# The recurrence of a three-part layer, from chunks of 128 tokens with scores of a whole chunk to sub-chunks of 64 with a running softmax

## The chip, the cores and the metric

One core of one Trainium2 chip. The metric is the device time of one execution in microseconds. A plain run gives 465.87 us (median of three, 465.07 to 466.24).

## The reference, cut to what matters

Batch 4, 8 heads, 768 tokens, head dimension 48; then a soft mixture of 8 experts with 4 slots each over all 3072 tokens (model dimension 384, hidden 1024), then a dense layer 384 to 2048 to 384 with a squared ReLU.

```python
    for t in range(S):
        kt, vt, rt = (k[:, :, t], v[:, :, t], r[:, :, t])
        cur = np.einsum('bhd,bhe->bhde', u[None] * kt, vt)
        y[:, :, t] = np.einsum('bhd,bhde->bhe', rt, state + cur)
        state = w[None, :, :, None] * state + np.einsum('bhd,bhe->bhde', kt, vt)
...
    logits = x @ phi
    d = logits - logits.max(0, keepdims=True)
    d = np.exp(d)
    d /= d.sum(0, keepdims=True) + 1e-09
    slot_input = d.T @ x
...
        h = np.maximum(slot_input[e] @ w1[e], 0.0)
        slot_out[e] = h @ w2[e]
...
    c = logits - logits.max(1, keepdims=True)
    c = np.exp(c)
    c /= c.sum(1, keepdims=True) + 1e-09
    return (c @ slot_out).astype(np.float32)
...
    h = x @ w_in
    r = np.maximum(h, 0.0)
    g = r * r
    return (g @ w_out).astype(np.float32)
```

## The kernel before

The program is written engine by engine: every engine has its own list, in an order written out by hand, and semaphores between them. There is no planner. All data is fp32; a matmul of fp32 stands in the trace as two records.

**Recurrence.** The tokens come in 6 chunks of 128 (`CH`), the heads in 4 pairs (`HP`), and a *unit* is one pair of heads in one chunk, for all 4 batches: 24 units. A pair of heads lies on partitions 0 to 47 and 64 to 111 (`HEAD_ROWS`). In each unit:

- VectorE multiplies the keys with powers of w (`keys`, L638), then the queries, each head on its own 48 partitions into a tile whose other half is zero (`queries`, L644, two instructions), so that one matmul over 112 rows gives the scores of both heads (L865: four matmuls, 256 columns). It carries the state on (`state`, L680), copies the scores above the diagonal over a prepared diagonal (`scores`, L667), sums the bonus term r·u·k (`bonus`, L662) and multiplies the keys in token-first layout (`keys_n`, L653).
- GpSimd makes the products r·k·u (`ruk`, L402, L405) and the diagonal matrices from `bonus` (`scores`, L413, 128x1024).
- TensorE makes scores (L865), output from state and scores (`y_ps`, L887 and L890, 16 matmuls of 128 columns) and the increment of the state (`aux_ps`, L904). In the second unit of a chunk it also does the router for the chunk before: logits (`pair_logits` L839, `token_logits` L854) and x turned to token-first (`turn_x`, L847).
- ScalarE copies out of PSUM (`copy_y` L474, `keep_x` L484, `state_in` L503).

All x (`x_sb`) and all logits are kept. The softmax over tokens comes after the recurrence: maximum of the first five chunks, exponentials, then the gather into slots (L948, 24 tiles), with the last chunk following and a factor that joins both.

**Experts** follow from L997 on (first layer; second layer L1022), then a short part up to `gin`, then the **dense layer**, 96 steps of 12 matmuls (L1081) with 384 columns. Weights come in through the SyncE queue: w1 in 24 pieces beside the recurrence, w2 after it.

The order on an engine is the order of its calls: for VectorE `scale`, `advance`, `mask_scores`, `sum_bonus`, `scale_n`; for TensorE `unit_scores`, `unit_output` of the unit before, `unit_state`.

## Time and profile before

| what | value |
|---|---|
| median of three runs | 465.87 us |
| span of the profiled execution | 464.3 us |
| PE busy | 405.0 us, 87% |
| VectorE busy | 331.9 us, 71% |
| ScalarE busy | 174.4 us, 38% |
| GpSimd busy | 153.1 us, 33% |
| DMA | 60.30 MB, mean 130 GB/s |
| first unit's scores on TensorE | at 11.65 us |
| last output of the recurrence | ends at 178.3 us |
| first matmul of the experts | at 190.56 us |
| dense layer in its steady rhythm | 237.4 to 464.3 us |

The profile is of one execution. Its own time beside the span isn't given apart; the median of the runs is 1.6 us above the span. Busy time of a pipelined engine like TensorE is not its capacity, so the stage must be found first (the windows), and then who is never idle in it.

### The profile page before, as it was taken

The page shows a single profiled execution, that of the slowest core. Times are in us where ns is not written, and L with a number is a line of the kernel's source. Part 1 is how long each engine was busy: PE and PEld are TensorE (multiplying, and loading weights), DVE is VectorE, ACT ScalarE, POOL GpSimd, SP SyncE. Part 2 cuts the span into 40 slices and gives each one's busy share as a digit, 9 for nine tenths or more (in the row PEclk, how much of TensorE's full clock was granted, in tenths as well). Part 3 has the DMA queues.
Part 4 walks back from the last instruction along what each step waited for, and adds up shares of the span by engine and source line. Part 5 has one row for each costly group of instructions (what it writes and reads, how often), then busy time and mean ns, then how long its engine had stood idle before and what let it go on. Part 6 is the DMA issues. An engine that isn't in the chain of part 4 may idle for free.

```text
span 464.3 us, 8783 instructions
## 1 busy us (share of the span) xinstructions
PE 405.0 (87%) x3096; PEld 349.0 (75%) x3096; DVE 331.9 (71%) x439; ACT 174.4 (38%) x312; POOL 153.1 (33%) x111
## 2 busy tenths in 40 slices
PE   0856968778787889999679999999999999999997
PEld 0544857657676766235279999999999999999997
DVE  8599999999999994611596565565556556556553
ACT  2011313123031314012535555555555555555552
POOL 6578878898888850110550000000000000000000
PEclk9957999999998989899889999999999999999999
DMA  6966667667666769999600010001001001001001
GB/s 174 243 195 193 202 206 218 183 201 231 194 196 203 225 238 316 373 373 403 212 0 1 1 68 2 1 1 68 0 0 68 0 0 68 0 0 68 1 0 68
DMA packets 31844, 60.30 MB, mean 130 GB/s; under 512 B 2640, under 2 KB 25296, under 8 KB 31440
## 3 DMA queue, kind: packets, MB, share of 16 engines
q1 hardware_dynamic: 31824, 60.02, 40.9%
q8 instruction: 13, 0.21, 0.2%
q14 instruction: 7, 0.06, 0.1%
HBM read 55.30 MB, written 4.72 MB: 129 GB/s over the span
## 4 chain that ended last, share of the span: by engine, by line
PE 61%; DVE 14%; POOL 10%; issue 5%; DVEq 1%; ACT 1%; POOLq 0%; ACTq 0%
PE out_ps L1081 43%; POOL scores L413 8%; PE h_ps L1059 5%; DVE scores L667 4%; DVE queries L644 4%; PE wide L997 3%; PE wide L1022 2%; PE score_ps L865 2%; DVE bonus L662 1%; DVE state L680 1%; PE y_ps L890 1%; POOL ruk L402 1%; POOL ruk L405 1%; PE wide L948 1%; DVE keys L638 1%
## 5 line engine op out<-in xcount | busy, mean ns | idle before, releaser
L1081 PE MATMUL out_ps<-w_hi,act_hi 128*128 128x384 f32 x384 | 130.5, 340 | 5.2 <-DVE act_lo L819 4.0
L1081 PE MATMUL out_ps<-w_hi,act_lo 128*128 128x384 f32 x384 | 131.0, 341 | 0.0
L1081 PE MATMUL out_ps<-w_lo,act_hi 128*128 128x384 f32 x384 | 130.5, 340 | 0.0
L814 DVE TENSOR_TENSOR act<-relu_h 128x512 f32<-128x512 f32 x96 | 68.2, 711 | 78.3 <-ACT relu_h L576 78.3
L576 ACT ACTIVATE relu_h<-h_ps 128x512 f32<-128x512 f32 x96 | 57.3, 597 | 100.6 <-PE h_ps L1059 97.9
L865 PE MATMUL score_ps<-queries,keys 112*128 112x256 f32 x192 | 60.5, 454 | 29.7 <-DVE queries L644 29.7
L413 POOL TENSOR_TENSOR scores<-ident,bonus 128x1024 f32<-128x1024 f32 x24 | 74.4, 3101 | 23.2 <-DVE bonus L662 23.2
L1081 PEld LDWEIGHTS out_ps<-w_hi,act_hi 128*128 128x128 f32 x384 | 72.7, 189 | 6.2 <-ACT act_hi L579 3.3
L1081 PEld LDWEIGHTS out_ps<-w_lo,act_hi 128*128 128x128 f32 x384 | 72.9, 190 | 3.8
L1081 PEld LDWEIGHTS out_ps<-w_hi,act_lo 128*128 128x128 f32 x384 | 72.5, 189 | 0.0
L819 DVE TENSOR_TENSOR act_lo<-act,act_hi 128x512 fp32r<-128x512 f32 x96 | 68.4, 713 | 4.6 <-ACT act_hi L579 1.0
L865 PEld LDWEIGHTS score_ps<-queries,keys 112*128 112x128 f32 x192 | 39.3, 222 | 41.8 <-DVE queries L644 24.1
L644 DVE TENSOR_TENSOR queries<-rk,q_pow 48x512 f32<-48x512 f32 x48 | 67.4, 1405 | 0.3
L579 ACT ACTIVATE act_hi<-relu_h 128x512 fp32r<-128x512 f32 x96 | 60.9, 634 | 3.9
L474 ACT ACTIVATE x_t<-y_ps 112x512 f32<-112x512 f32 x24 | 14.3, 597 | 111.2 <-PE y_ps L890 111.2
L890 PE MATMUL y_ps<-scores,rkv 128*48 128x128 f32 x384 | 38.0, 286 | 1.8 <-DVE scores L667 1.8
L1059 PE MATMUL h_ps<-mix_t,gin 128*128 (+1 forms) x96 | 38.0, 398 | 0.0
L887 PE MATMUL y_ps<-queries,state 112*48 112x128 f32 x320 | 32.6, 278 | 4.3 <-DVE scores L667 4.1
L667 DVE COPY_PREDICATED scores<-mask,score_ps 128x1024 f32<-128x1024 uint32 x24 | 32.0, 1333 | 4.8 <-POOL scores L413 4.8
L402 POOL TENSOR_TENSOR ruk<-rkv 128x384 f32<-128x384 f32 x24 | 31.0, 1291 | 10.8 <-DMA rkv<-in_rkv_n 8.5
L890 PEld LDWEIGHTS y_ps<-scores,rkv 128*48 128x48 f32 x384 | 24.6, 129 | 4.3 <-DVE scores L667 2.9
L887 PEld LDWEIGHTS y_ps<-queries,state 112*48 112x48 f32 x320 | 18.6, 123 | 10.8 <-issue 7.5
(145 smaller groups left out, 369.1 us busy)
## 6 DMA issues: line engine op xcount, KB each, us to landing
rkv<-in_rkv_n SPq DMA_DIRECT2D x24, 576.0 KB, 4.6
rk<-in_rk_t SPq DMA_DIRECT2D x48, 192.0 KB, 3.2
w_sb<-in_w SPq DMA_DIRECT2D x24, 384.0 KB, 5.1
w_room<-in_w SPq DMA_DIRECT2D x4, 1536.0 KB, 11.1
out_dram<-y_sb SPq DMA_DIRECT2D x5, 768.0 KB, 3.5
w_x<-in_w SPq DMA_DIRECT2D x2, 1536.0 KB, 14.0
w_w<-in_w SPq DMA_DIRECT2D x4, 768.0 KB, 11.5
w_in_sb<-in_w_in SPq DMA_DIRECT2D x3, 1024.0 KB, 13.0
```

The source lines that it names most:

```text
L413: nc.gpsimd.tensor_tensor(scores[hp % 2][:, :, :, :].rearrange("p b h t -> p (b h) t"), ident[:, :].unsqueeze(1).broadcast_to([P, 2 * B, P ...
L576: nc.scalar.activation(relu_h[f % 2][:, :], h_ps[f % 4][:, :], ACT.Relu).then_inc(relu_done, 1)
L579: nc.scalar.activation(act_hi[f % 4][:, :], relu_h[f % 2][:, :], ACT.Square).then_inc(act_hi_done, 1)
L644: last = nc.vector.tensor_tensor(queries[hp][rows, :, half], rk[hp % 2][rows, 0], q_pow[rows, hp].unsqueeze(1).broadcast_to([D, B, P]), AL ...
L667: nc.vector.copy_predicated(scores[hp % 2][:, :, :, :].rearrange("p b h t -> p (b h) t"), mask[:, :].unsqueeze(1).broadcast_to([P, 2 * B, P]),
L814: nc.vector.tensor_tensor(act[f % 2][:, :], relu_h[f % 2][:, :], relu_h[f % 2][:, :], ALU.mult).then_inc(act_done, 1)
L819: nc.vector.tensor_tensor(act_lo[f % 4][:, :], act[f % 2][:, :], act_hi[f % 4][:, :].bitcast(F32), ALU.subtract).then_inc(act_lo_done, 1)
L865: last = nc.tensor.matmul(score_ps[hp % 2][:, 2 * P * b:2 * P * (b + 1)], keys[hp % 2][0:PAIR, b], queries[hp][0:PAIR, b].rearrange("p h t ...
L887: nc.tensor.matmul(y_ps[SECOND * half:SECOND * half + D, cols], state[0:PAIR, hp, b], queries[hp][0:PAIR, b, half], start=True, stop=False)
L890: last = nc.tensor.matmul(y_ps[SECOND * half:SECOND * half + D, cols], rkv[hp][:, 2, b, D * half:D * (half + 1)], scores[hp % 2][:, b, hal ...
L1059: nc.tensor.matmul(h_ps[f % 4][:, :], gin[:, P * f:P * (f + 1)], mix_t[:, bass.ds(g * B, B), :], start=True, stop=True).then_inc(h_mm, 1)
L1081: last = nc.tensor.matmul(out_ps[t][:, 0:DM], a[f % 4][:, tok], w[:, f], start=(f == 0 and i == 0), stop=(f == NF - 1 and i == 2))
```

## The change

The recurrence is written anew and the router is folded into it.

- **Sub-chunks.** A chunk of 128 tokens is two sub-chunks of 64 (`SUBS`), each with its own scores. Keys, queries and values use one half of the array's rows and one half of its columns per matmul: a score matmul reads 48 rows (one head) and 64 key columns, and streams 128 columns: 64 of the queries and 64 of a second set. Sixteen of them make a unit. The state has two versions per unit: `state_a` at the middle of the first sub-chunk, `state_b` at the second (powers of w count from the middle, token 64).
- **Powers.** VectorE multiplies the keys of both heads in one instruction (`times_keys`), GpSimd the queries in one (`times_queries`). The zero-filled queries are gone.
- **Diagonal.** The second set, queries times u·w (ScalarE, `second_queries`), gives the bonus on its diagonal; a second masked copy takes it (`mask_scores`, masks `strict` and `diag`). The GpSimd products, the diagonal matrices and the sum are gone.
- **Keys in token-first layout** aren't loaded and multiplied, but turned from `keys` by TensorE (`turn_keys`) and copied by ScalarE (`copy_keys`). Of the token-first load only the values stay (192 KB for 576).
- **Router.** Logits are made slot-first per chunk (`slot_logits`), the softmax over tokens runs along with a running negative maximum (`new_peaks`, `exponents`), p and logits are turned (`turn_logits`), and the gather of each chunk goes into an accumulator that is rescaled (`gather`, `gathered`). `x_sb` holds one chunk. After the recurrence only the last chunk's share is left, and a factor per batch and slot (`GAIN`, `fold_g`).
- **Weights.** All of w1 and two experts of w2 come in beside the recurrence; four experts of w2 after it instead of six.
- The experts' matmuls and the dense layer are as before, but for where tiles lie; on VectorE one clearing of PSUM (`wide[1]`) moves behind `slot_t`.

Cut to its core:

```diff
-            def scale(c, hp):
-                n = HP * c + hp
-                ve.wait_ge(rk_in[hp % 2], 32 * (2 * c + hp // 2 + 1))
-                wait(ve, score_done, n - 1)
-                nc.vector.tensor_tensor(keys[hp % 2][0:PAIR], rk[hp % 2][0:PAIR, 1],
-                                        k_pow[0:PAIR, hp].unsqueeze(1).broadcast_to([PAIR, B, P]), ALU.mult)
-                wait(ve, y_done, n - 3)
-                if isinstance(c, int) and c == 0:
-                    ve.wait_ge(q_cleared, hp + 1)
-                for half, rows in enumerate(HEAD_ROWS):
-                    last = nc.vector.tensor_tensor(queries[hp][rows, :, half], rk[hp % 2][rows, 0],
-                                                   q_pow[rows, hp].unsqueeze(1).broadcast_to([D, B, P]), ALU.mult)
-                last.then_inc(qk_done, 1)
...
-            def mask_scores(hp):
-                nc.vector.copy_predicated(scores[hp % 2][:, :, :, :].rearrange("p b h t -> p (b h) t"),
-                                          mask[:, :].unsqueeze(1).broadcast_to([P, 2 * B, P]),
-                                          score_ps[hp % 2][:, :].rearrange("p (a t) -> p a t", t=P)
-                                          ).then_inc(mask_done, 1)
...
+            def times_keys(c, hp):
+                n = HP * c + hp
+                ve.wait_ge(rk_in[hp], 32 * (c + 1))
+                wait(ve, score_mm, n - 3)
+                nc.vector.tensor_tensor(keys[hp][0:PAIR], rk[0:PAIR, hp, 1],
+                                        powers[0:PAIR, 1, hp, 1:P + 1].unsqueeze(1).broadcast_to([PAIR, B, P]),
+                                        ALU.mult).then_inc(k_done, 1)
...
+            def times_queries(c, hp):
+                n = HP * c + hp
+                pool.wait_ge(rk_in[hp], 32 * (c + 1))
+                wait(pool, y_mm, n - 3)
+                nc.gpsimd.tensor_tensor(
+                    queries[0:PAIR, hp // 2, hp % 2], rk[0:PAIR, hp, 0].rearrange("p b (j t) -> p b j t", t=SUB),
+                    powers[0:PAIR, 0, hp, 0:P].rearrange("p (j t) -> p j t", t=SUB).unsqueeze(1).broadcast_to([PAIR, B, 2, SUB]),
+                    ALU.mult).then_inc(q_done, 1)
...
+            def mask_scores(c, hp):
+                n = HP * c + hp
+                ve.wait_ge(const_step, MASKS)
+                ve.wait_ge(score_mm, n + 1)
+                wait(ve, y_mm, n - 1)
+                parts = score_ps[:, :].rearrange("p (a k t) -> p a k t", k=2, t=SUB)
+                into = scores[hp % 2][:, :, :, :].rearrange("p h b t -> p (h b) t")
+                nc.vector.copy_predicated(into, strict[:, :].unsqueeze(1).broadcast_to([P, 2 * B, SUB]), parts[:, :, 0]
+                                          ).then_inc(mask_half, 1)
+                ve.wait_ge(const_step, MASKS)
+                ve.wait_ge(mask_half, n + 1)
+                nc.vector.copy_predicated(into, diag[:, :].unsqueeze(1).broadcast_to([P, 2 * B, SUB]), parts[:, :, 1]
+                                          ).then_inc(masked, 1)
...
+            def new_peaks(c):
+                ve.wait_ge(lg_done, c + 1)
+                wait(ve, p_done, c)
+                nc.vector.reduce_max(PEAK, lg_sb[:, :], AX.X).then_inc(peak_step, 1)
+                ve.wait_ge(peak_step, 3 * c + 1)
+                nc.vector.scalar_tensor_tensor(NEW_PEAK, PEAK, -1.0, OLD_PEAK, ALU.mult, ALU.min).then_inc(peak_step, 1)
+                ve.wait_ge(peak_step, 3 * c + 2)
+                nc.vector.tensor_tensor(STEP, NEW_PEAK, OLD_PEAK, ALU.subtract).then_inc(peak_step, 1)
+                ve.wait_ge(peak_step, 3 * c + 3)
+                nc.vector.tensor_copy(OLD_PEAK, NEW_PEAK).then_inc(peak_done, 1)
...
+            def unit_scores(c, hp):
+                n = HP * c + hp
+                pe.wait_ge(const_step, IDENT)
+                pe.wait_ge(q2_done, n + 1)
+                wait(pe, masked, n)
+                both = slice(0, 3, 2) if hp < 2 else slice(1, 3)
+                for b in range(B):
+                    for j in range(2):
+                        for h in range(2):
+                            last = nc.tensor.matmul(
+                                score_ps[SUBS[j], BANK * h + P * b:BANK * h + P * (b + 1)],
+                                keys[hp][head_rows(h), b, SUBS[j]], queries[head_rows(h), both, hp % 2, b, j],
+                                start=True, stop=True)
+                last.then_inc(score_mm, 1)
...
+            def within(hp, j, b, x):
+                h = x ^ (b % 2)
+                nc.tensor.matmul(into_y(j, x, b), vals[hp][SUBS[j], b, D * h:D * (h + 1)], scores[hp % 2][SUBS[j], h, b],
+                                 start=(b == 0), stop=False, skip_group_check=True)
+            def from_state(hp, j, b, h):
+                state = state_b[head_rows(h), b] if j else state_a[head_rows(h), hp, b]
+                return nc.tensor.matmul(into_y(j, h ^ (b % 2), b), state, queries[head_rows(h), hp // 2, hp % 2, b, j],
+                                        start=False, stop=False, skip_group_check=True)
...
+            def output_front(c, hp):
+                n = HP * c + hp
+                pe.wait_ge(const_step, IDENT)
+                pe.wait_ge(masked, n + 1)
+                pe.wait_ge(b_done, n + 1)
+                wait(pe, ya_done, n)
+                wait(pe, yb_done, n)
+                if not isinstance(c, int) or c > 0:
+                    pe.wait_ge(a_done, n - HP + 1)
+                for b in range(B):
+                    for x in range(2):
+                        within(hp, 1, b, x)
+                        within(hp, 0, b, x)
+                for b in range(B):
+                    if not isinstance(c, int) or c > 0:
+                        from_state(hp, 0, b, 0)
+                    last = from_state(hp, 1, b, 1)
+                last.then_inc(y_front, 1)
...
+            def gather(parts):
+                for cols, part in zip((slice(0, XHALF), slice(XHALF, XC)), parts):
+                    for b in range(B):
+                        last = nc.tensor.matmul(part[SLOTS * b:SLOTS * (b + 1)], disp[:, SLOTS * b:SLOTS * (b + 1)],
+                                                x_sb[:, b, cols], start=True, stop=True)
+                last.then_inc(gather_mm, 1)
...
+            def chunk(c, first):
+                last_chunk = isinstance(c, int) and c == CH - 1
+                for hp in range(HP):
+                    n = HP * c + hp
+                    unit_state(c, hp, None if first else {1: lg_done, 2: acc_done}.get(hp))
+                    if not (last_chunk and hp == HP - 1):
+                        unit_scores(*later(c, hp, 1))
+                    output_front(c, hp)
+                    if hp == 0 and not first:
+                        slot_logits(range(HP)).then_inc(lg_mm, 1)
+                    if not (last_chunk and hp + 2 >= HP):
+                        turn_keys(*later(c, hp, 2))
+                    if hp == 1 and not first:
+                        if not last_chunk:
+                            pe.wait_ge(end_done, n + 1)
+                        pe.wait_ge(p_done, c)
+                        turn_logits().then_inc(turn_mm, 1)
+                    if not first or hp > 0:
+                        turn_x(n - 1, (hp - 1) % HP)
+                    if hp == 1 and not first:
+                        pe.wait_ge(logits_done, c)
+                        pe.wait_ge(x_done, HP * c)
+                        gather((spare_a[:, 0:XHALF], spare_b[:, 0:XC - XHALF]))
+                    output_back(c, hp)
```

TensorE in the loop over the chunks, before (state increment of one unit, scores of the next, and the first batch of the output of four; `x8` counts matmuls):

```order
L904 MATMUL aux_ps<-rkv_65,keys_n_71 48x48 x8
L862 REGISTER_ALU
L865 MATMUL score_ps<-queries_62,keys_58 128x256 x4
L882 REGISTER_ALU
L887 MATMUL y_ps<-queries_61,state 48x128 x2
L890 MATMUL y_ps<-scores_73,rkv_65 48x128 x2
```

and one unit of the change at the same place, up to the transposes:

```order
L930 MATMUL inc_ps<-vals_65,keys_n_69 48x48 x16
L911 MATMUL score_ps<-queries,keys_61 64x128 x16
L950 MATMUL y_ps<-scores_67,vals_65 48x64 x16
L955 MATMUL y_ps<-queries,state_a 48x64
L955 MATMUL y_ps<-queries,state_b 48x64
L955 MATMUL y_ps<-queries,state_a 48x64
L955 MATMUL y_ps<-queries,state_b 48x64
L955 MATMUL y_ps<-queries,state_a 48x64
L955 MATMUL y_ps<-queries,state_b 48x64
L955 MATMUL y_ps<-queries,state_a 48x64
L955 MATMUL y_ps<-queries,state_b 48x64
L899 MATMUL turn_ps<-ident,keys_58 128x112 x4
```

A unit had 4 score matmuls of 256 columns, 16 output matmuls of 128 and 8 state matmuls of 48; it now has 16 of 128, 32 of 64 (eight of them after the transposes) and 16 of 48, and four transposes of keys in every unit.

VectorE, one unit in the loop before:

```order
L638 TENSOR_TENSOR keys_59<-rk_57,k_pow 112x512
L52 REGISTER_ALU
L644 TENSOR_TENSOR queries_61<-rk_57,q_pow 48x4x128 x2
L680 SCALAR_TENSOR_TENSOR state<-state,w_88,state_in_75 112x192
L667 COPY_PREDICATED scores_72<-mask,score_ps 128x1024
L660 REGISTER_ALU
L662 TENSOR_REDUCE bonus_80<-ruk_69 128x8
L653 TENSOR_TENSOR keys_n_71<-rkv_65,kn_pow 128x384
```

and now:

```order
L709 COPY x_t<-y_ps 112x4x64
L722 TENSOR_TENSOR state_b<-inc_ps,state_a 112x192
L727 TENSOR_TENSOR state_end_75<-inc_ps,state_b 112x192
L736 COPY_PREDICATED scores_68<-strict,score_ps 128x512
L740 COPY_PREDICATED scores_68<-diag,score_ps 128x512
L55 REGISTER_ALU
L696 TENSOR_TENSOR keys_59<-rk,powers 112x512
```

The queries, the bonus sum and the token-first keys have left VectorE; half of the copy of y has come to it.

## Rows read from the trace of the kernel before

**Rows 1.** Windows, by stretch: span, busy us (records) of PE, PEld, DVE, ACT, POOL, clock, DMA share, GB/s.

```profile
16.50:99.00 82.50, 60.18 (x628) 48.30 (x630) 77.02 (x81) 14.90 (x35) 66.48 (x38) 0.90 0.72 204
99.00:178.40 79.40, 65.42 (x795) 54.05 (x791) 76.12 (x83) 18.38 (x43) 60.81 (x32) 0.96 0.68 212
178.40:190.50 12.10, 10.45 (x95) 5.55 (x95) 5.72 (x14) 4.18 (x10) 1.62 (x8) 1.00 1.06 376
190.50:237.40 46.90, 40.62 (x325) 18.97 (x325) 20.57 (x27) 15.97 (x26) 12.91 (x15) 0.89 0.82 299
237.40:464.30 226.90, 222.72 (x1232) 218.24 (x1232) 138.18 (x202) 118.39 (x197) 1.55 (x1) 1.00 0.06 21
```

**Rows 2.** Chain that ended last, shares of the span (the page).

```profile
PE out_ps L1081 43%; POOL scores L413 8%; PE h_ps L1059 5%; DVE scores L667 4%; DVE queries L644 4%; PE wide L997 3%; PE wide L1022 2%; PE score_ps L865 2%; DVE bonus L662 1%; DVE state L680 1%; PE y_ps L890 1%; POOL ruk L402 1%; POOL ruk L405 1%; PE wide L948 1%; DVE keys L638 1%
```

**Rows 3.** Timeline, VectorE, one steady unit: start us, us, line, tiles, count.

```profile
106.13 0.69 DVE L638 TENSOR_TENSOR keys<-rk,k_pow 112x512 f32<-112x512 f32 x1
106.73 2.98 DVE L644 TENSOR_TENSOR queries<-rk,q_pow 48x512 f32<-48x512 f32 x2
109.74 1.04 DVE L680 SCALAR_TENSOR_TENSOR state<-state,w,state_in 112x192 f32<-112x192 f32 x1
110.71 1.33 DVE L667 COPY_PREDICATED scores<-mask,score_ps 128x1024 f32<-128x1024 uint32 x1
111.93 0.54 DVE L662 TENSOR_REDUCE bonus<-ruk 128x8 f32<-128x384 f32 x1
112.39 0.55 DVE L653 TENSOR_TENSOR keys_n<-rkv,kn_pow 128x384 f32<-128x384 f32 x1
```

**Rows 4.** Timeline, GpSimd, the same unit.

```profile
105.83 3.33 POOL L413 TENSOR_TENSOR scores<-ident,bonus 128x1024 f32<-128x1024 f32 x1 [0.92 <-DVE bonus L662]
```

**Rows 5.** Timeline, TensorE's weight loads, the same stretch.

```profile
105.00 0.55 PEld L847 LDWEIGHTS x_ps<-ident,x_t 112*128 112x128 f32 x4
105.50 0.30 PEld L865 LDWEIGHTS score_ps<-queries,keys 112*128 112x128 f32 x2
105.83 0.55 PEld L847 LDWEIGHTS aux_ps<-ident,x_t 112*128 112x128 f32 x4
106.33 0.97 PEld L854 LDWEIGHTS lg_ps<-fold,logits_t 128*128 128x128 f32 x8
107.43 0.17 PEld L887 LDWEIGHTS y_ps<-queries,state 112*48 112x48 f32 x4
...
109.12 0.51 PEld L904 LDWEIGHTS aux_ps<-rkv,keys_n 128*48 128x48 f32 x16
109.76 1.59 PEld L865 LDWEIGHTS score_ps<-queries,keys 112*128 112x128 f32 x8
```

**Rows 6.** Timeline, weight loads of the first expert layer.

```profile
195.26 0.11 PEld L997 LDWEIGHTS wide<-w_sb,slot_t 128*4 128x4 f32 x4 [0.32 <-issue]
195.69 0.11 PEld L997 LDWEIGHTS wide<-w_sb,slot_t 128*4 128x4 f32 x4 [0.32 <-issue]
```

**Rows 7.** Timeline, start of the recurrence: GpSimd and TensorE.

```profile
7.56 1.47 POOL L432 TENSOR_TENSOR kn_powt<-w_pow 112x512 f32<-112x512 f32 x1 [0.21 <-DVE w_inv L618]
11.65 3.78 PE L865 MATMUL score_ps<-queries,keys 112*128 112x256 f32 x8 [1.50 <-DVE queries L644]
```

**Rows 8.** Groups of instructions, by form: busy us, mean ns, idle before.

```profile
L474 ACT ACTIVATE x_t<-y_ps 112x512 f32<-112x512 f32 x24 | 14.3, 597 | 111.2 <-PE y_ps L890 111.2
L630 DVE COPY kn_pow<-lg_ps 128x192 f32<-128x192 f32 x2 | 0.7, 352 | 0.0
L778 DVE COPY out_t<-wide 128x384 f32<-128x384 f32 x1 | 0.6, 558 | 8.1 <-PE wide L1034 8.1
```

**Rows 9.** Timeline, last copy of the recurrence, first matmul of the experts.

```profile
178.33 0.60 ACT L474 ACTIVATE x_t<-y_ps 112x512 f32<-112x512 f32 x1 [1.88 <-PE y_ps L890]
190.56 7.45 PE L997 MATMUL wide<-w_sb,slot_t 128*4 128x512 f32 x51 [0.40 <-issue]
```

**Rows 10.** DMA from 20 to 170 us: bytes moved and mean rate.

```profile
DMA packets 14941, 31.43 MB, mean 210 GB/s; under 512 B 1397, under 2 KB 9700, under 8 KB 14933
```

More of the change, by code:

```diff
@@ L22 @@
 XC = DM + 1
+XHALF = 193
 E, SLOTS, FE = 8, 32, 1024
@@ L52, in wait, with count_ahead, later @@
         eng.wait_ge(semaphore, value)
+def count_ahead(eng, c, low, high, low_next, high_next):
+    for i in range(low, high):
+        eng.to_reg(HP * c + i)
+    for i in range(low_next, high_next):
+        eng.to_reg(HP * (c + 1) + i)
+def later(c, hp, ahead):
+    q = hp + ahead
+    while q >= HP:
+        q -= HP
+        c = c + 1
+    while q < 0:
+        q += HP
+        c = c - 1
+    return c, q
 def program(nc, rk_t, rkv_n, w_t, u, phi, w1, w2, w_in, w_out, out):
@@ new lines, in unit_state @@
+            def unit_state(c, hp, spare_read):
+                n = HP * c + hp
+                pe.wait_ge(const_step, IDENT)
+                if spare_read:
+                    pe.wait_ge(spare_read, c)
+                pe.wait_ge(kt_done, n + 1)
+                pe.wait_ge(vals_in[hp], 16 * (c + 1))
+                wait(pe, b_done, n)
+                if not (isinstance(c, int) and c == CH - 1 and hp > 0):
+                    wait(pe, end_done, n)
+                for b in range(B):
+                    for h in range(2):
+                        for j in range(2):
+                            last = nc.tensor.matmul(
+                                inc_ps[head_rows(h), BANK * j + D * b:BANK * j + D * (b + 1)],
+                                keys_n[hp % 2][SUBS[j], b, h], vals[hp][SUBS[j], b, D * h:D * (h + 1)],
+                                start=True, stop=True)
+                last.then_inc(inc_mm, 1)
@@ L940, in _ @@
-            for b in range(B):
-                turn_x(CH - 1, b, [x_ps, y_ps])
-            token_logits(CH - 1)
-            def gather(tiles, bank, first, last_tile):
-                for i in tiles:
-                    q = i % QUADS
-                    last = nc.tensor.matmul(bank[SLOTS * q:SLOTS * (q + 1), 0:XC], disp[:, i], x_sb[:, i],
-                                            start=(i < first + QUADS), stop=(i >= last_tile - QUADS))
-                return last
-            earlier = wide[2][:, BANK:2 * BANK]
@@ L964, in _ @@
-            gather(range(4 * QUADS, EARLIER), earlier, 0, EARLIER)
-            pe.wait_ge(lag_exp, 1)
-            nc.tensor.matmul(wide[3][:, BANK:BANK + 1], fold4[0:SLOTS, :], small[0:SLOTS, 45:46], start=True, stop=True
-                             ).then_inc(lag_mm, 1)
-            pe.wait_ge(disp_done, 2)
-            gather(range(EARLIER, TILES), wide[2], EARLIER, TILES).then_inc(slot_mm, 1)
-            pe.wait_ge(slot_in_done, 1)
+            chunk(CH - 1, False)
+            slot_logits(range(HP - 1))
```

893 lines of the change are left out of this document (447 added, 446 removed).

## The prediction

> **What bounds the kernel now.** I read the windows first, because each stage has its own limit. From 237.4 us to the end TensorE runs the dense layer without a pause (222.7 of 226.9 us); the change doesn't touch it. From 190.5 to 237.4 the experts follow, also the same matmuls [rows 1]. So only what lies before 190.5 us can move. In the recurrence VectorE is busy for 77.0 of 82.5 us and 76.1 of 79.4 us, TensorE for 60.2 and 65.4. The chain names GpSimd's diagonal matrices (L413) beside VectorE's lines [rows 2], but GpSimd idles ahead of each of them until VectorE's `bonus` is there [rows 4]; the chain goes through both because they meet once per unit. VectorE's own timeline shows the period: keys start at 106.13, the next keys at 112.85, 6.72 us later, and the six instructions of a unit stand end to end: 0.69 + 2.98 + 1.04 + 1.33 + 0.54 + 0.55, with overlaps of some tenths [rows 3]. 24 units at 6.72 are 161 us of the 178.3 us until the last output [rows 9]. The reader should see that TensorE's share here (0.75 to 0.8 busy) says little: it waits for VectorE's queries, then hurries.
>
> **VectorE after the change.** The queries (2.98), the sum (0.54), token-first keys (0.55) and the long state update (1.04) leave. What it has per unit: keys 0.69; two masked copies of 512 for one of 1024 at 1.33, so half of it plus a start each, 0.73 x 2 [rows 3]; copy of 256 columns of y, between 0.35 (192 columns) and 0.56 (384), 0.42 [rows 8]; two additions of 192 columns out of PSUM, 0.35 each by the same row. That is 3.3 us, and per chunk a maximum, three tiny steps and two rescalings, about 1.7 us, 0.4 per unit: **3.7 us**. ScalarE gets five copies per unit, none over 512 columns, which cost it at most 0.60 each [rows 8]: 3.0 us, 3.3 with the router's. GpSimd has one product of 112x512, 1.47 us in the head [rows 7]. None of the three is the bound if TensorE needs more, and they are hidden behind it. Queries are three units ahead, keys three, transposes two, so their latencies have cover; if TensorE were faster than 3.7 us, VectorE would be next.
>
> **TensorE after the change**, record by record (two records per matmul), at its full rate:
> - State increment: 32 records of 48 columns. Before, 16 of them load their weights in 0.51 us [rows 5]; less the length of one load (0.12 of it) that is 26 ns a record: 0.83 us.
> - Output: 64 records of 64 columns. The row shows 26 ns for 48 columns and, for 128 columns, 32 records from 107.43 to 109.12, 53 ns [rows 5]. I take 26: streaming 64 columns in two column halves would be 27 by halving 53. Both ways give **1.7 us**, as much as the 16 wide matmuls cost. Nothing is gained here.
> - Scores: 32 records of 128 columns, four tiles of the array at once. In the expert layer four records in four column strips, 512 columns each, repeat every 0.43 us, 107 ns a record [rows 6]; for 128 columns that is 27 ns: 0.87 us. The upper bound is the y row's 53 ns (two tiles at once): 1.7 us. I take 27, since the four tiles write different columns or banks; no row shows halves of the rows at work together. Before: 1.59 us.
> - Transposes: 4 of keys (new) and 4 of x. Four records and two score records repeat every 0.83 us; less two score records of 0.2 it is 0.10 us a record [rows 5]: 16 records, 1.6 us.
> - Router per chunk: 32 records at 27 ns, 4 turning records at 0.11 (L854, 8 in 0.97), 16 gather records of 193 columns at 40 ns (193/512 of 107): 1.95 us, 0.5 per unit. The old router leaves.
> - Changes between kinds of tiles, two to three per unit. From the last load of L854 (its eight end at 107.30) to the next kind at 107.43 the gap is 0.13 [rows 5]; 0.3 per unit, between 0 and 0.6.
> - Waits: in the second unit TensorE waits for ScalarE to copy the turned exponents, then the third for VectorE's rescaling. About 0.5 each, 0.25 per unit, between 0.1 and 0.5.
>
> Sum 0.83 + 1.7 + 0.87 + 1.6 + 0.5 + 0.3 + 0.25 = **6.0 us** for 6.72: TensorE becomes the bound, and the gain in the loop is small although VectorE loses 3 us. The same number of half-size matmuls is where it goes. The own bounds are 5.4 (no gaps) and 6.5.
>
> The Trainium skill speaks against such a cut: TensorEngine Tiling (Array Packing), Performance Considerations, says that a matmul carries about 60 cycles of overhead and that the tiling factor shouldn't be taken from a dimension already small. At 2.4 GHz that is an estimate of 25 ns, and 64 output records would cost 1.6 us rather than the 0.85 us that four tiles at once would stream; the 48-column row agrees with the floor at 26 ns. The same page, Key Properties, says that a change of tiling mode drains the engine; no length is given.
>
> **Head.** The powers are ready at about 7.4 us before [rows 7]; now there are two sets, some 0.9 us more. GpSimd then multiplies (1.5), ScalarE makes the second set (0.6), scores at the low rate take 1.7, so the first state matmul is at about 12.7 us. In the first chunk a unit has 16 records fewer and no router: 4.85 us; the low rate of the first 4 us costs 3 us (eight score records take 3.78 for 1.59 [rows 5, 7]), one transpose set is missing (-0.8): the chunk ends at 12.7 + 21.6 = 34.3 us. Twenty units at 6.0, less 2.5 for scores and transposes that the last two units don't have: **151.8 us** for 178.3, a gain of 26.5.
>
> **Tail to the experts.** Before it is 12.2 us (178.33 to 190.56 [rows 9]): logits, two maxima over partitions, 24 gathers. Now: copy of y 0.6, last logits 0.5, copy 0.4, maximum and three steps 1.2, exponentials 0.7, turning 0.6, copy 0.4, gather 0.9, rescaling 1.0, fold 1.0, copy and start 0.7: **8.0 us**, a gain of 4.2. The column maximum per slot (`top`, `GAIN`) runs beside it.
>
> **DMA** stays hidden: a unit moves 1.37 MB as before (values for three tensors, but w1 in larger pieces), at 6.0 us 230 GB/s; 210 is the mean now [rows 10] and 376 is reached in the tail [rows 1]. In the tail two experts of w2 fewer are to come. I give the stretch to 237.4 nothing: its loads come a few us earlier, which may spare GpSimd's late rounding some collision with VectorE (0 to 2 us).
>
> Sum: 26.5 + 4.2 = 30.7 off the span of 464.3; off the median of the runs, 1.6 above the span, it gives **435 us**.
>
> **Rivals.**
> - *Two tiles at once, not four.* Scores cost 53 ns a record, 0.85 us more per unit, T = 6.8: 435 + 24 x 0.85 = **455 us**. For it: no row shows two halves of the rows together. Against it: four column strips do work together [rows 6]. Other waits of this size (a unit of VectorE's chain that isn't covered) come to the same. Chance 0.2.
> - *TensorE falls to its low rate.* The clock was 0.90 and 0.96 in the recurrence [rows 1], with pauses of over a microsecond before each unit's scores; in the head a score record costs 0.47 for 0.20 [rows 5, 7]. At the low rate a unit of the change is 10 us, 4 us more. TensorE being the bound, this counts in full. From 8 units of 24 at the low rate the gain is gone; at half of them: 435 + 12 x 4 = **483 us**, slower. For it: a quarter of a unit is now transposes and the rest small matmuls. Against it: TensorE would have no long pause, and between 99 and 178 us, where a quarter of the units had dense transposes, the clock was higher, not lower. Chance 0.12. The Trainium skill has a rule for it: TensorE: Matmul & The Clock Gate, Part 4, says that transposes don't count as the engine being busy as other matmuls do. This trace doesn't bear it out.
> - *Faster than forecast* (T near 5.4, the experts' part gains 2 us): **419 us**. Chance 0.07.
> - *Nothing moves*: a wait that I don't see (PSUM of scores has one buffer now) ties a unit to 6.7 and the head is later: within 0.3% of before. Chance 0.03.
>
> **How the numbers follow.** The forecast, T from 5.7 to 6.4 (428 to 445 us), has 0.58. Range: 424 to 460 us, which takes in most of the first rival; what is left out is the low clock, a part of the fastest case and the same. A measurement tells 0.3%, 1.4 us, from no change. Faster: 0.58 + 0.19 + 0.07 = 0.84, taken down to 0.82; same 0.03; slower 0.15.
>
> **What would show it.** Right: in the recurrence TensorE is busy almost throughout with hardly an idle entry, VectorE for some 60%; a period of L911 near 6.0 us; 16 records of L911 apart by 27 ns; last L955 near 150 us; the first expert matmul 8 us after it. Two tiles at once: L911's loads span 1.7 us. Low clock: granted clock under 0.8 between 20 and 150 us and L899 at 0.19 a record. Wrong in kind: TensorE idle for more than 1 us per unit behind one of `masked`, `b_done`, `kt_done`.

## The result, and the profile after

The change takes 426.6 us (median of five, 418.53 to 429.94) where the kernel before takes 465.87. The ratio, formed from undisturbed executions only (of the change 418.53 and 424.52), is 0.9042, 95% interval 0.8965 to 0.9118: some 45 us less where 31 were forecast. 0.9042 of 465.87 is 421 us (418 to 425 by the interval), below the range of 424 to 460, though not by much: the median of all five lies inside it, and the change timed once more (below) gave 0.9105, which is 424 us. The profile is of the execution of 418.53 us: its span is 416.8, against 464.3 before.

| | before | forecast | after |
|---|---|---|---|
| first state matmul | – | 12.7 | 13.5 |
| last output ends | 178.3 | 151.8 | 137.6 |
| from there to the first expert matmul | 12.2 | 8.0 | 9.4 |
| from there to the end | 273.7 | 273.7 | 269.8 |

So 40.7 of the 47.5 us by which the span is shorter come from the recurrence and what stands ahead of it. The page of the change: busy times, instruction queue, chain (answers to [rows 2]).

```profile
PE 375.1 (90%) x5068; PEld 333.8 (80%) x5068; DVE 251.9 (60%) x440; ACT 195.8 (47%) x374; POOL 53.7 (13%) x69
...
q8 instruction: 21, 0.34, 0.4%
...
PE 87%; issue 4%; DVE 3%; DMA 2%; ACT 1%; SPq 1%; POOL 0%; DVEq 0%; ACTq 0%
PE out_ps L1168 48%; PE score_ps L911 7%; PE h_ps L1148 5%; PE y_ps L955 4%; PE y_ps L950 3%; PE turn_ps L899 3%; PE inc_ps L930 3%; PE wide L1088 3%; PE wide L1112 3%; PE x_ps L941 2%; DMA rk<-in_rk_t 2%; PE inc_ps L993 1%; PE inc_ps L1004 1%; DVE acc L760 1%; PE wide L1099 1%
```

GpSimd's 8% and VectorE's lines of the recurrence have left the chain but for the rescaling (`acc`, 1%), TensorE's own lines stand in their place: it is the bound now. `issue` (4%) is time in which an engine waited for nothing that the profile shows.

The windows of the change, cut near the chunks' starts (within 0.6 us), with the columns of [rows 1]:

```profile
13.30:39.90 26.60, 22.04 (x496) 19.66 (x490) 13.61 (x25) 8.17 (x17) 5.83 (x8) 0.91 1.02 275
39.90:66.00 26.10, 19.25 (x594) 16.79 (x588) 14.63 (x31) 10.28 (x27) 5.17 (x5) 0.89 0.72 209
66.00:84.66 18.66, 17.15 (x595) 15.32 (x595) 13.90 (x30) 9.69 (x26) 4.90 (x5) 0.91 0.89 246
84.66:101.66 17.00, 15.64 (x595) 13.74 (x595) 13.80 (x30) 9.48 (x26) 4.67 (x5) 1.00 1.06 295
101.66:118.80 17.14, 16.29 (x635) 14.41 (x639) 13.79 (x30) 9.72 (x26) 4.38 (x4) 1.00 1.06 282
118.80:137.60 18.80, 15.48 (x526) 13.45 (x521) 9.83 (x21) 5.90 (x17) 1.28 (x1) 0.91 0.61 202
137.60:147.00 9.40, 6.70 (x69) 4.34 (x73) 3.12 (x12) 2.43 (x9) 0.31 (x1) 0.68 0.99 333
```

Two things are to be seen. The chunks of the settled loop (the rows from 84.66 and 101.66) last 17.0 us or a little less, 4.25 us a unit, where 6.0 was forecast. And the same 590 records of TensorE last 26.1 us in chunk 1. The chunks' own lengths, from state matmul to state matmul, are 26.0, 26.5, 18.7, 17.0, 16.5 and, to the last output, 19.4.

TensorE's timeline in the settled loop, the start of a unit (start us, us, line, shape, count, idle before):

```profile
101.66 0.57 PE L930 MATMUL inc_ps<-vals,keys_n 64*48 64x48 f32 x31 [0.59 <-issue]
...
102.06 1.06 PE L911 MATMUL score_ps<-queries,keys 48*64 48x128 f32 x31
102.91 0.66 PE L950 MATMUL y_ps<-scores,vals 64*48 64x64 f32 x32
...
103.72 1.08 PE L993 MATMUL inc_ps<-x_t,phi_sb 112*32 112x128 f32 x32
104.74 0.60 PE L899 MATMUL turn_ps<-ident,keys 112*128 112x112 f32 x4
105.17 0.26 PE L941 MATMUL x_ps<-ident,x_t 112*128 112x112 f32 x1
105.27 0.26 PE L941 MATMUL x_ps<-swap,x_t 112*128 112x112 f32 x1
```

Read from start to start, since each group's last record ends some 0.2 us after the next has begun. 32 state records take 0.36 us (101.66 to 102.02, where L911 begins), 11 ns each; 32 score records 0.89 us, 28 ns; the 48 output records in front 0.70, 14.5 ns (the 16 in the back, behind the transposes, take 0.37 with the gap at the change of kind); the four transposes of keys 0.43, those of x 0.10 each. And the transposes are **four records, not eight**: L899 counts 96 in the whole trace, 24 units by four transposes. The row before already had it: `L847 ... x4` is one call of `turn_x`, which writes four transposes [rows 5].

VectorE in the same unit, which answers to [rows 3]:

```profile
102.29 0.36 DVE L722 TENSOR_TENSOR state_b<-inc_ps,state_a 112x192 f32<-112x192 f32 x1 [0.65 <-PE inc_ps L930]
102.68 0.36 DVE L727 TENSOR_TENSOR state_end<-inc_ps,state_b 112x192 f32<-112x192 f32 x1
103.23 0.73 DVE L736 COPY_PREDICATED scores<-strict,score_ps 128x512 f32<-128x512 uint32 x1 [0.19 <-PE score_ps L911]
104.07 0.75 DVE L740 COPY_PREDICATED scores<-diag,score_ps 128x512 f32<-128x512 uint32 x1
104.70 0.68 DVE L696 TENSOR_TENSOR keys<-rk,powers 112x512 f32<-112x512 f32 x1
```

The durations are those forecast, 3.45 us a unit (13.8 of 17.0), and VectorE now waits for TensorE. GpSimd's group in the whole trace (busy us, mean ns, idle before): it too waits for TensorE, and 1.23 us of 4.25 is all it does.

```profile
L429 POOL TENSOR_TENSOR queries<-rk,powers 112x512 f32<-112x512 f32 x24 | 29.5, 1231 | 81.2 <-PE y_ps L955 76.9
```

What makes the first chunks long shows in the chain of waits from 10 to 150 us (start us, us, what):

```profile
15.57 1.99 PE score_ps L911 x32
...
28.85 1.49 issue
...
35.43 1.83 issue
...
45.41 0.48 PE inc_ps L930 x26
45.88 2.26 issue
48.14 0.30 PE inc_ps L930 x5
48.44 1.39 PE score_ps L911 x32
...
54.14 1.08 issue
...
58.62 0.90 issue
...
61.95 1.84 issue
...
65.40 0.63 issue
...
83.95 0.71 issue
```

The 2.26 us stand in the middle of a group: 26 records of `unit_state`, a pause, five more, with no wait written between them. From 66.0 to 118 the only such entries left are those of 0.6 to 0.7 us that stand at the loop's return (at 83.95 and 101.07). Chunk 0 and chunk 5 have such pauses too (28.85 and 35.43 above, 1.95 at 128.36). Chunks 0, 1 and 5 have one thing in common: their instructions are run for the first time. Chunk 0 and 5 are written out, chunk 1 is the loop's first pass.

The trace has the instruction queue's packets, of 16 KB each, and they fit. From 13.5 to 62.5 us there are eight, and in the 55 us of the settled loop behind them (62.5 to 118) one:

```profile
q8 instruction: 1, 0.02, 0.1%
```

And each pause above has its packet: the one of the pause at 45.88 moves from 45.5 to 46.8, and TensorE goes on at 48.1. All seven pauses of 0.9 us and more from 28.85 to 128.36 end 1.3 to 1.5 us after a packet has landed, and each packet took 1.0 to 1.4 us.

A second loss goes with the pauses. TensorE's granted clock was at its lower level (0.5 of the full one) in five short stretches between 31.7 and 134 us: from 31.7, 38.5, 48.8, 65.9 and 130.7. Each begins 0.4 to 2.1 us after the end of one of the five pauses of 1.49 us and more; after those of 1.08 and 0.90 none follows. The groups from 48.44 to 52.05 take 3.6 us, where the same ones take 2.2 later (72.44 to 74.63): some 1.4 us a stretch. Before 28 us the clock column is no guide, since it says 1.00 where no record of the clock is there; the score records tell the low level by themselves, 1.99 us for 32 at 15.57 where it is 0.90 later, and TensorE's records keep that length until 28.1.

### The profile page after: what moved, and what is told of

Its sections match the earlier page's. It is cut to its first block, busy times and chain, and to the rows that moved or that the text cites. A ratio compares the mean times of both kernels' runs of the same rounds, so it can differ in the third digit from the quotient of the medians.

```text
span 416.8 us, 12693 instructions
## 1 busy us (share of the span) xinstructions
PE 375.1 (90%) x5068; PEld 333.8 (80%) x5068; DVE 251.9 (60%) x440; ACT 195.8 (47%) x374; POOL 53.7 (13%) x69
## 4 chain that ended last, share of the span: by engine, by line
PE 87%; issue 4%; DVE 3%; DMA 2%; ACT 1%; SPq 1%; POOL 0%; DVEq 0%; ACTq 0%
PE out_ps L1168 48%; PE score_ps L911 7%; PE h_ps L1148 5%; PE y_ps L955 4%; PE y_ps L950 3%; PE turn_ps L899 3%; PE inc_ps L930 3%; PE wide L1088 3%; PE wide L1112 3%; PE x_ps L941 2%; DMA rk<-in_rk_t 2%; PE inc_ps L993 1%; PE inc_ps L1004 1%; DVE acc L760 1%; PE wide L1099 1%
## 5 line engine op out<-in xcount | busy, mean ns | idle before, releaser
L429 POOL TENSOR_TENSOR queries<-rk,powers 112x512 f32<-112x512 f32 x24 | 29.5, 1231 | 81.2 <-PE y_ps L955 76.9
L911 PE MATMUL score_ps<-queries,keys 48*64 48x128 f32 x768 | 34.2, 320 | 1.2 <-POOL fold L439 1.2
L911 PEld LDWEIGHTS score_ps<-queries,keys 48*64 48x64 f32 x768 | 27.9, 162 | 2.0 <-POOL fold L439 1.4
L736 DVE COPY_PREDICATED scores<-strict,score_ps 128x512 f32<-128x512 uint32 x24 | 17.7, 735 | 13.3 <-PE score_ps L911 13.0
L899 PE MATMUL turn_ps<-ident,keys 112*128 112x112 f32 x96 | 16.4, 300 | 9.8 <-POOL swap L423 8.3
L930 PE MATMUL inc_ps<-vals,keys_n 64*48 64x48 f32 x768 | 16.9, 227 | 8.7 <-issue 6.8
L955 PE MATMUL y_ps<-queries,state_b 48*48 48x64 f32 x384 | 23.0, 236 | 0.0
L950 PE MATMUL y_ps<-scores,vals 64*48 64x64 f32 x768 | 18.9, 237 | 3.9 <-issue 3.3
L930 PEld LDWEIGHTS inc_ps<-vals,keys_n 64*48 64x48 f32 x768 | 14.2, 137 | 10.2 <-issue 9.9
L955 PE MATMUL y_ps<-queries,state_a 48*48 48x64 f32 x320 | 18.1, 225 | 3.8 <-issue 3.8
```

The lines of the kernel that those rows point to most:

```text
L429: nc.gpsimd.tensor_tensor(queries[0:PAIR, hp // 2, hp % 2], rk[0:PAIR, hp, 0].rearrange("p b (j t) -> p b j t", t=SUB), powers[0:PAIR, 0, ...
L899: last = nc.tensor.transpose(turn_ps[:, P * b:P * b + PAIR], keys[hp][0:PAIR, b], ident[0:PAIR, 0:PAIR])
L911: last = nc.tensor.matmul(score_ps[SUBS[j], BANK * h + P * b:BANK * h + P * (b + 1)], keys[hp][head_rows(h), b, SUBS[j]], queries[head_row ...
L930: last = nc.tensor.matmul(inc_ps[head_rows(h), BANK * j + D * b:BANK * j + D * (b + 1)], keys_n[hp % 2][SUBS[j], b, h], vals[hp][SUBS[j], ...
L950: nc.tensor.matmul(into_y(j, x, b), vals[hp][SUBS[j], b, D * h:D * (h + 1)], scores[hp % 2][SUBS[j], h, b], start=(b == 0), stop=False, sk ...
L955: return nc.tensor.matmul(into_y(j, h ^ (b % 2), b), state, queries[head_rows(h), hp // 2, hp % 2, b, j], start=False, stop=False, skip_gr ...
```

## The experiments

All were timed beside the kernel before on the same chip. A chunk's length is taken from its logits matmuls (L993) to the next chunk's; for the change that gives 26.6, 17.1, 17.0, 16.5 and 17.3 us for chunks 1 to 5, the groups standing at 43.0, 69.6, 86.7, 103.7, 120.2 and 137.5.

**State increments twice.** Is a small record paid for by its columns over the tiles at work, 10 ns, or by a floor of 26?

```diff
-                for b in range(B):
+                for b in list(range(B)) * 2:
```

(in `unit_state`; the second set writes the same sums again.)

> Each state increment matmul is issued twice (the second overwrites the first with the same values): 32 records of 48 columns more per unit. Theory (TensorE is the bound in the loop, four tiles of the array work at once, a record costs its streaming over four, 11 ns as in the trace of the change): a chunk in the loop goes from 17.0 to about 18.5 us, the whole 8 to 9 us slower. Rival of the prediction (a floor of 26 ns a record): 0.83 us per unit, 20 us slower. Rival that VectorE, ScalarE or the transfers set the period: no change beyond 2 us.

Measured: 437.32 us (436.13 to 441.61), 0.9398 of before (0.9319 to 0.9476). TensorE's timeline in the loop:

```profile
118.75 0.93 PE L930 MATMUL inc_ps<-vals,keys_n 64*48 64x48 f32 x63
119.47 0.28 PE L911 MATMUL score_ps<-queries,keys 48*64 48x128 f32 x1
```

64 records in 0.72 us, 11 ns each. The loop's chunks are 18.6, 18.3 and 17.7 us, 1.3 more than the change's, 0.33 per unit: 10 ns for each of the 32 records added. The floor of 26 would be 3.3 us a chunk. But the whole is 11 us slower by the medians and 14 to 17 by the ratios, not 8 to 9: chunk 1 took 32.9 us, the last 22.2, with pauses of 3.24 and 4.11 us (41.75, 139.84) where the change has 2.26 and 1.95. The extra cost lies where instructions run for the first time, and this kernel has more of them (24 packets for 21).

**The same rows in a row.** Is it the alternating halves of rows that makes scores cheap?

```diff
-                for b in range(B):
-                    for j in range(2):
-                        for h in range(2):
+                for h in range(2):
+                    for b in range(B):
+                        for j in range(2):
```

> The same 16 score matmuls per unit, but all eight of one head (one half of the array's rows) before all eight of the other, so that only the two column halves can alternate. Theory (all four tiles work at once when neighbours differ in rows and columns): a score record goes from 28 ns to about 53 ns, 0.8 us more per unit, 19 us in the whole. Rival (halves of the rows never work together, the gain is from the columns alone): scores stay at 0.90 us per unit and the time stays within 2 us.

Measured: 431.61 us (428.9 to 432.73), 0.9253 (0.9191 to 0.9315). TensorE's timeline in the loop:

```profile
108.59 0.28 PE L911 MATMUL score_ps<-queries,keys 48*64 48x128 f32 x1
...
108.63 1.44 PE L911 MATMUL score_ps<-queries,keys 48*64 48x128 f32 x29
...
109.91 0.22 PE L950 MATMUL y_ps<-scores,vals 64*48 64x64 f32 x1
```

The 32 records now take 1.32 us, 42 ns each for 28, and a chunk of the loop 18.3 to 18.9. So neighbours in different halves of rows do work together, and the order of the loops in `unit_scores` is worth 1.7 us a chunk, and in the whole some 5 us by the medians and 7 to 10 by the ratios. It is not the 53 ns and the 19 us that two tiles alone would make; why it stops at 42 no run here tells.

**The loop written out.** If the pauses come from instructions that arrive late, every chunk must become like chunk 1.

```diff
-            with pe.Fori(1, CH - 1) as c:
-                count_ahead(pe, c, 1 - HP, HP + 1, -1, 3)
-                pe.to_reg(16 * (c + 1))
+            for c in range(1, CH - 1):
                 chunk(c, False)
```

> TensorE's loop over chunks 1 to 4 is written out, nothing else: same instructions in the same order, but each chunk's code is new. Theory (the pauses in the middle of a group of matmuls, seen in chunks 0, 1 and 5 and not in passes three and four of the loop, are TensorE waiting for instructions that it hasn't had yet): chunks 3 and 4 go from 17 us to 20 to 26 us and the whole gets 8 to 25 us slower; the pause at the loop's return (0.6 to 0.7 us) goes. Rival (pauses come from late data or from the low clock at the start): chunks 3 and 4 stay at 17 us, the whole within 2 us or 2 us faster.

Measured: 454.24 us (452.41 to 456.76), 0.9737 (0.9663 to 0.981): 28 us slower than the change, by nothing but copies of the same code, and more than the 25 that were expected at most. The windows of chunks 2 to 4 and the last:

```profile
71.00:97.00 26.00, 19.98 (x602) 17.49 (x596) 12.62 (x28) 9.79 (x25) 4.76 (x4) 0.81 0.76 197
97.00:125.00 28.00, 21.98 (x594) 18.82 (x586) 14.03 (x32) 9.78 (x25) 4.79 (x4) 0.76 0.75 221
125.00:151.00 26.00, 19.30 (x615) 16.49 (x610) 13.52 (x29) 9.66 (x25) 4.74 (x4) 0.87 0.47 132
151.00:174.00 23.00, 15.25 (x446) 12.37 (x442) 8.85 (x20) 5.52 (x16) 0.00 (x0) 0.83 0.42 139
```

From the page and from the timeline of TensorE's weight loads:

```profile
q8 instruction: 36, 0.59, 0.6%
...
89.04 0.49 PEld L930 LDWEIGHTS inc_ps<-vals,keys_n 64*48 64x48 f32 x19 [4.18 <-issue]
```

The instruction queue moved 36 packets instead of 21, each of 16 KB: 15 for three more copies of the body, five per chunk. A chunk uses them up in 17 us when they are there (one in 3.4 us), and takes 23 to 28 when they must be fetched; from 66.6 to 147.9 us there are 15, one in 5.4 us. The pause of 4.06 us at 84.98 has a packet from 86.15 to 87.6, landed 1.4 us before its end. The entry at the loop's return is gone, as expected. The clock falls behind the pauses, to 0.76 in one window, which adds to them: where the same body is looped it holds 1.00. This settles the kind of the loss. The Trainium skill, Runtime: NRT & Kernel Launch, Instruction fetch mechanics, has the blocks of 16 KiB, and this trace agrees (0.59 MB in 36 packets); but it calls the fetch hidden by the time that instructions take, and advises to unroll since a taken branch stalls. Here it is the other way: the branch costs 0.6 us a chunk, the unrolled body 6 to 11 in chunks 2 to 5. The measurement decides: with records of 11 to 28 ns the engine outruns the fetch.

**The same edit in the kernel before**, where TensorE waits for VectorE.

```diff
-            with pe.Fori(2, CH) as c:
+            for c in range(2, CH):
```

> The kernel before, with TensorE's loop over chunks 2 to 5 written out. Theory (late instructions cost what no other engine covers): before the change TensorE needs 28 matmuls per unit of 6.7 us and waits for VectorE anyway, so new code for every chunk is fetched in its shadow: within 0.5% of the kernel before, where the same step cost the changed kernel 28 us. Rival (a written-out loop costs TensorE the same pauses in either kernel): 10 us or more slower.

Measured: 466.99 us, 1.0017 of before (0.9987 to 1.0047). The queue moved 20 packets for 13, seven for three more copies, and a chunk of 27 us needs one in 11.5 us. Nothing is lost in the time; whether no instruction came late or TensorE's waits for VectorE covered it, this run doesn't separate. Either way the kernel before had no such loss to show, and the loss is new with the change.

**Weights after the recurrence.** Do the weight transfers slow TensorE, the fetch, or neither? All of w1 and the two early experts of w2 come behind the last output.

```diff
-                if hp >= 2:
-                    load_w1(0, hp - 2)
...
-                    load_w1(2 * c - 1 + hp // 2, hp % 2)
...
+            sp.wait_ge(y_mm, UNITS - 1)
+            for p in range(2 * E):
+                load_w1(p // 2, p % 2)
+            for p in range(2 * W2_EARLY):
+                load_w2(p // 2, p % 2)
```

> All of w1 and the two early experts of w2 are loaded after the last output but one of the recurrence instead of beside it, 15.7 MB. Theory (instruction loads are late because they queue among the weight transfers): the mid-group pauses shrink to under 0.5 us each, chunks 0 and 1 go from 26 us each to 18 to 21, the last output from 137.6 to 115 to 125 us. Rival one (instruction fetch is slow by itself): pauses stay at 1 to 2 us and the last output near 135 us. Rival two (steady chunks are bound by transfers, which fill 1.06 of the engines there): chunks 3 and 4 fall under 16 us. The whole gets slower by 15 to 35 us, since the experts then wait for w1.

Measured: 443.47 us (439.02 to 447.56), 0.9472, the experts starting at 157.55. But the recurrence ends at 126.6 instead of 137.6. Its windows by chunk:

```profile
13.50:33.90 20.40, 17.70 (x476) 15.65 (x470) 13.31 (x25) 7.17 (x17) 6.06 (x8) 1.00 0.66 163
33.90:57.20 23.30, 16.96 (x603) 14.52 (x602) 14.61 (x31) 10.66 (x29) 5.20 (x5) 1.00 0.38 105
...
74.30:91.20 16.90, 15.59 (x594) 13.66 (x594) 13.75 (x30) 9.46 (x26) 4.65 (x5) 1.00 0.53 141
```

The settled chunks are what they were (17.1, 16.9) although the DMA share there fell from 1.06 to 0.53: the loop isn't bound by transfers. Chunks 0 and 1 lose 5.6 and 3.2 us of their length, and the last output, expected at 125 at the latest, comes at 126.6. The pauses are still 0.59 to 1.56 us where under 0.5 was expected, and this is a miss: the fetch is slow by itself, the first of the rivals. A packet takes 0.9 to 1.5 us here as there, and TensorE goes on 1.3 to 1.5 us after it.

What shortens the two chunks is mostly the other loss. The window from 28 to 40 us, in the change and here:

```profile
28.00:40.00 12.00, 8.68 (x218) 7.60 (x215) 5.56 (x10) 3.58 (x8) 1.18 (x2) 0.80 0.96 254
28.00:40.00 12.00, 9.78 (x331) 8.30 (x329) 8.53 (x19) 5.71 (x16) 3.02 (x3) 1.00 0.47 130
```

The pauses of chunks 0 and 1 sum to 6.9 us for 9.4, but the records of TensorE have their low-clock length in 8 us of the two chunks instead of 22, and from 23.8 us on the full level holds until 123. Half of those 14 us would be 7 at the most (an estimate), the pauses give 2.5, and the chunks are 8.8 us shorter. Why the full level comes earlier and holds here, though pauses of up to 1.56 us stand in these chunks too, no run tells.

**The change again**, for the spread.

> The change itself once more, as the mark for the two beside it: 418 to 430 us. Its spread comes from the pauses of chunks 0, 1 and 5, so between runs those chunks should differ by a few us and chunks 3 and 4 by under 0.5 us.

Measured: 426.36 us (421.67 to 431.29), 0.9105 (0.9056 to 0.9154). The chain in chunk 1:

```profile
40.00 0.11 PE y_ps L950 x6
40.10 4.89 issue
44.99 0.98 PE y_ps L950 x25
```

The same code paused for 4.89 us here and nowhere for as long in the first profile (its packet moves only from 42.2 to 43.6); the later passes are 17.1 and 17.0 us long, as before. Executions of one kernel differ in the first passes.

**Queries on VectorE as well**, nothing in the loop on GpSimd: what is the help of GpSimd worth?

```diff
-                nc.gpsimd.tensor_tensor(
+                nc.vector.tensor_tensor(
                     queries[0:PAIR, hp // 2, hp % 2], rk[0:PAIR, hp, 0].rearrange("p b (j t) -> p b j t", t=SUB),
```

(`times_queries` moves into VectorE's list behind `times_keys`; two waits on the constants of the start are added.)

> The queries of both heads are multiplied by VectorE after the keys, GpSimd does nothing in the recurrence. VectorE is busy 13.8 of 17.0 us in a chunk of the loop; four products of 0.7 us make it 16.6. Theory (TensorE is the bound, VectorE has just that much room): chunks 3 and 4 stay between 17 and 18 us, the whole 0 to 6 us slower than the change. Rival (GpSimd's share is what makes the change fast, as VectorE bound the kernel before): chunks at 19 us or more, 10 us or more slower.

Measured: 423.55 us (422.03 to 430.97), 0.9064 (0.9032 to 0.9096). A settled chunk of it, window and VectorE's timeline:

```profile
70.46:88.11 17.65, 15.88 (x597) 13.82 (x594) 15.67 (x34) 9.82 (x25) 0.00 (x0) 0.99 0.89 230
...
99.99 0.68 DVE L685 TENSOR_TENSOR queries<-rk,powers 112x512 f32<-112x512 f32 x1
```

The product costs VectorE 0.68 us where the kernel before spent 2.98 on its zero-filled queries [rows 3]; VectorE is busy for 15.7 of 17.7 us and the loop's chunks are 17.7 to 18.2 us, 0.5 to 1.6 us longer. In the whole the two can't be told apart. Of the 2.98 us taken off VectorE, 2.3 are the shape of the queries, one instruction on all 112 partitions for two on 48; that GpSimd does the rest is worth about 1 us a chunk. Why one of the old instructions took twice as long as the new one for as many columns isn't tested.

**w1 from chunk 2 on.** The weights keep away from chunk 0 and the start of chunk 1 (SyncE runs ahead: the first piece is issued between 42 and 46 us), and all of w1 still comes before the last output.

```diff
-            with sp.Fori(1, CH - 2) as c:
+            with sp.Fori(2, CH - 2) as c:
...
-                    load_w1(2 * c - 1 + hp // 2, hp % 2)
+                    load_w1(2 * c - 4 + hp // 2, hp % 2)
```

(and the early loads of w2 behind the others.)

> w1 comes in from chunk 2 on, one half expert per unit to the last unit, nothing of it beside chunks 0 and 1; the first experts of w2 follow the recurrence. Theory (instruction loads queue behind weight transfers, and the loop's later passes need none): chunk 0 takes 20 to 22 us for 26, chunk 1 about 23 for 26.5, chunks 3 and 4 stay at 17, w2 still comes in time; the whole 5 to 9 us faster than the change. Rival (the weights only move the pauses to chunk 5, or w2 is then late): within 2 us of the change.

Measured: 423.57 us (417.14 to 425.6), 0.896 (0.8916 to 0.9003), beside 426.36 and 0.9105 (0.9056 to 0.9154) for the change on the same chip. It is the fastest kernel here, 3 us by the medians and 7 by the ratios; beside the first timing of the change (0.8965 to 0.9118) the intervals touch. Its logits of chunks 1 and 2 stand 3 to 7 us earlier than in the two profiles of the change (39.75 and 65.20, for 43.0 to 46.4 and 68.7 to 69.6), but its last chunk takes 23 us, with pauses of 2.09, 1.68 and 1.60, and the clock at 0.76 there. 5 to 9 us were expected, so the gain is borne out weakly, and its theory (instruction loads queue behind the weights) is not: the pauses at 19.62 and 37.35, before any weights move, are of 3.70 and 1.60 us. Chunk 0 is shorter all the same (22.3 us for 26.0), as with the weights after the recurrence.

## Why the prediction was wrong, point by point

- **Where the bound goes: right.** TensorE became the bound of the settled loop, VectorE's 3.7 us a unit measured 3.45, GpSimd and ScalarE are hidden, DMA too (with the weights away the settled chunks stay at 17 us).
- **Output, "Nothing is gained here": the first step that failed.** I took 26 ns a record from 48-column state loads that stood on all 128 rows and could use two tiles at a time [rows 5]. With halves of rows and of columns four work, and 64 columns cost 14.5 ns. All 64 records take 1.07 us (0.70 and 0.37), 0.6 less than forecast. The Trainium skill's overhead of about 60 cycles a matmul (TensorEngine Tiling, Performance Considerations), by my estimate 25 ns, which I set against each record, isn't borne out as a floor per record: 11 ns is the start-to-start distance of the 48-column records over four tiles, and the doubled state confirms it. For a matmul of two records that is 22 ns, and whether a single tile has such a floor no run shows. The row agreed with the estimate by chance: two tiles would make twice 11.
- **State increment, 0.83:** 0.36, 0.47 less, by the same error.
- **Transposes, 1.6:** 0.8. I counted two records for each, as for the other matmuls of the recurrence. The row showed four records for four transposes. The 0.10 us a record was right.
- **Scores, 0.87:** 0.89, by the row of the expert layer [rows 6]. The rival of two tiles fell; the run with one half of rows after the other shows what it would have been like, at half the price (0.43 us a unit more for 0.85).
- **Router, 1.95 a chunk:** 1.0 for the logits (L993), 0.9 for the gather (L1004) and 0.2 for the turning: 2.1.
- **Waits, 0.25 a unit:** one of 0.62 us a chunk, behind the rescaling (110.75 to 111.38), so 0.16 a unit.
- The three errors (output, state, transposes) make 1.9 of the 6.0 us; the rest is 4.1 where 4.25 was measured, the loop's return of 0.6 us a chunk being the difference.
- **What I didn't have at all, the late instructions.** With the terms mended, chunk 0 would last 14.4 us (21.6 less 4 x 1.8) and the last output would end at 12.7 + 14.4 + 20 x 4.25 - 1.8 = 110 us. Measured is 137.6. The 27 us lie at: start 0.8, chunk 0 11.6, chunk 1 9.5, chunk 2 1.7, last chunk 4.2, less 0.5 in chunk 4, which has no return. In chunk 1 the pauses are 6.1 (the 0.6 of the return belongs to every pass) and two stretches of low clock some 2.8: 8.9 of 9.5. In chunk 2 it is one stretch, 1.4 of 1.7; in the last chunk one pause and one stretch, 3.4 of 4.2. In chunk 0 the pauses are 3.3 and a stretch behind them 1.4; the rest is largely the low rate at the start, for which I had put 4 us and which held until 28.1, and a wait of 1.24 us for GpSimd (at 14.33); these weren't measured apart. The errors had opposite signs, so 435 came closer than its steps, by luck: the terms made the last output 42 us too late (151.8 for 110), what was missing 27 too early.
- **The low clock as a rival:** it came in part, in chunks 0 to 2 and in the last. Transposes didn't bring it: with a fifth of each unit for them the loop holds 1.00, so the Trainium skill's rule on them (TensorE: Matmul & The Clock Gate, Part 4) isn't seen here either. After 28 us it came where TensorE had just stood still for instructions.
- **Tail, 8.0:** 9.4, at a granted clock of 0.68, with one pause of 0.65 us (140.19). No run was made for it.
- **After the first expert matmul, 0 to 2 us:** 3.9. GpSimd's rounding of the dense weights ends 46.2 us after it instead of 48.4; that would be 2.2 of them. This wasn't tested.

TensorE at 146.98, the row that answers to [rows 9]:

```profile
146.98 1.89 PE L1088 MATMUL wide<-w_sb,slot_t 128*4 128x512 f32 x8 [0.35 <-DVE slot_t L806]
```

**Still open:** why TensorE stays at the low rate until 28 us in the change and reaches the full one at 24 without the weights; why the last chunk is long when w1 starts later; what makes the packets come late although each moves in 1.0 to 1.4 us; and what brings the 3.9 us at the end.

## What to carry to other kernels

Price a small matmul by its columns over the number of tiles that its neighbours leave free to work at once, and take it from start to start of a group with the same rows and columns; count the records of an operation in a row before you multiply. When a change makes an engine's instructions short, ask whether they arrive in time: in a loop they do after the first pass, written out they may not, and the sign is a pause with no releaser in the middle of a group, with a packet of the instruction queue just before its end. Count the low clock behind it as a second loss. Two large errors can cancel in the total, so compare each stage, and not the end alone.

## What the runs showed of the hardware that was unexpected

- Four tiles of half the rows by half the columns: 11 ns (48 columns), 14.5 ns (64), 28 ns (128) a record. With the same rows in neighbours: 42 ns for 28.
- A transpose of fp32 is one record (96 of L899 for 96 transposes), the fp32 matmuls of state, scores and output are two each (768 of L911 for 384).
- TensorE's code comes in packets of 16 KB, five for the 600 matmul records of a chunk and their loads. Used up in 3.4 us each, they come one in 5.4 (15 in 81 us, loop written out), with pauses of 0.6 to 4.9 us; needed every 11.5 us, they cost no time. A pause ends 1.3 to 1.5 us after its packet has landed, in seven of seven cases of the change and in the six of chunks 0 and 1 without the weights. Weights beside them don't show in the packets (0.9 to 1.5 us either way).
- Behind a stop of TensorE the granted clock can fall, and costs again: five pauses of 1.5 to 2.3 us in the change were each followed by a short stretch at the lower level, some 1.4 us of loss each; those of 0.9 and 1.1 us weren't, nor was one of 1.56 us in the run with the weights later.
- The return of the loop costs 0.5 to 0.7 us in every pass.
